# Splitting the weights once per layer, short GpSimd pieces, and a softplus correction without GpSimd

## The reference

```python
kv = np.einsum('bhsd,bhse->bhde', k, v)          # batch 4, heads 8, 576 tokens, 64
out = np.einsum('bhsd,bhde->bhse', q, kv)
rms = np.sqrt(np.mean(out * out, axis=-1, keepdims=True) + 1e-06)
x = (out / rms * g_norm)                         # then as 2304 tokens x 512

h = x @ w_in                                     # 512 x 2048
g = h * (1.0 / (1.0 + np.exp(-1.702 * h)))       # layer 1
x = g @ w_out                                    # 2048 x 512

h = x @ w_in2
g = np.maximum(h, 0.0) + np.log1p(np.exp(-np.abs(h)))   # layer 2: softplus
y = g @ w_out2
```

## Time and profile before

| | us |
|---|---|
| median of 3 runs | 1026.78 (1023.02 to 1027.03) |
| the profiled execution | 1023.06 |
| its span, first to last instruction | 1021.3 |
| mean granted clock of PE | 0.931 of 2.4 GHz |
| PE busy | 868.1 (85%) |
| DVE busy | 698.9 (68%) |
| POOL busy | 540.9 (53%) |
| ACT busy | 433.8 (42%) |
| DMA | 53.28 MB, mean 52 GB/s |

### The profile page before, as it was taken

How to read it: one execution, slowest core, us unless ns; L and a number is a source line. 1 busy time by engine, 2 the same in 40 slices (tenths; PEclk the granted TensorE clock), 3 DMA queues, 4 the chain that set the end, 5 groups by cost and what they waited for, 6 DMA issues and landing times.

```text
span 1021.3 us, 12292 instructions
## 1 busy us (share of the span) xinstructions
PE 868.1 (85%) x4584; PEld 774.1 (76%) x4584; DVE 698.9 (68%) x1029; ACT 433.8 (42%) x751; POOL 540.9 (53%) x416
## 2 busy tenths in 40 slices
...
DMA packets 22219, 53.28 MB, mean 52 GB/s; under 512 B 2064, under 2 KB 7824, under 8 KB 22160
## 3 DMA queue, kind: packets, MB, share of 16 engines
...
q10 hardware_dynamic: 576, 0.33, 0.1%
...
## 4 chain that ended last, share of the span: by engine, by line
DVE 36%; PE 35%; ACT 10%; POOL 8%; issue 7%; DMA 3%; DVEq 0%; POOLq 0%; ACTq 0%
PE ps L514 19%; DVE gs_f L879 9%; PE ps L553 8%; POOL fix L378 8%; DVE gs_f L848 5%; PE ps L556 4%; ACT gs L675 4%; DVE gs L883 4%; DVE xs L812 3%; DVE xs_f L801 3%; DVE gs_f L856 3%; PE ps L559 3%; DVE fix L867 3%; DVE gs_f L875 2%; DMA kv_in_sb<-k_v 2%
## 5 line engine op out<-in xcount | busy, mean ns | idle before, releaser
L514 PE MATMUL ps<-xs,w_in 128*128 128x384 f32 x2016 | 443.1, 363 | 126.1 <-DVE gs_f L848 111.8
L514 PEld LDWEIGHTS ps<-xs,w_in 128*128 128x128 f32 x2016 | 380.8, 205 | 161.3 <-issue 101.5
L357 POOL TENSOR_TENSOR w_in<-w_in_f,w_in 128x1024 fp32r<-128x1024 f32 x96 | 217.2, 2268 | 75.4 <-ACT w_in L680 75.2
L559 PE MATMUL ps<-w_out,gs 128*128 128x512 f32 x864 | 234.0, 409 | 9.0 <-DVE gs L883 8.7
L378 POOL TENSOR_TENSOR fix<-ex,fix 128x384 f32<-128x384 f32 x96 | 111.5, 1161 | 216.8 <-DVE fix L867 216.8
L553 PE MATMUL ps<-gs,w_out 128*128 128x512 f32 x576 | 209.1, 396 | 0.0
L559 PEld LDWEIGHTS ps<-w_out,gs 128*128 128x128 f32 x864 | 168.4, 199 | 43.8 <-issue 16.0
L848 DVE TENSOR_TENSOR gs_f<-ps,gs_f 128x384 f32<-128x384 f32 x240 | 130.8, 550 | 90.6 <-PE ps L514 89.1
L556 PE MATMUL ps<-gs,w_out 128*128 128x256 f32 x576 | 162.8, 283 | 0.0
L879 DVE TENSOR_TENSOR gs_f<-gs_f,fix 128x384 f32<-128x384 f32 x96 | 96.5, 1005 | 61.8 <-POOL fix L378 61.1
L883 DVE TENSOR_TENSOR gs<-gs_f,gs 128x384 fp32r<-128x384 f32 x96 | 91.2, 950 | 52.4 <-ACT gs L675 50.1
...
## 6 DMA issues: line engine op xcount, KB each, us to landing
w_in_f<-w_in SPq DMA_DIRECT2D x48, 512.0 KB, 3.3
kv_in_sb<-k_v SPq DMA_DIRECT2D x16, 512.0 KB, 8.7
w_out_f<-w_out SPq DMA_DIRECT2D x16, 512.0 KB, 4.1
...
tail_sb<-k_v SPq DMA_DIRECT2D x3, 256.0 KB, 11.8
...
```

The source lines that it names most:

```text
L357: nc.gpsimd.tensor_tensor(w[:, LO, slots], w_in32[:, n % W_BUFS, LO, slots], w[:, HI, slots].bitcast(F32), ALU.subtract).then_inc(w_split, 1)
L514: mm = nc.tensor.matmul(ps[:, bank, 0:HALF], w[:, wp, W_OF[k], cols], xs[:, k, xp, t], start=(new and t == 0 and (wp, xp) == (HI, HI)), st ...
L559: mm = nc.tensor.matmul(ps[:, ACC_BANK + j, 0:DM], g[:, j * P:(j + 1) * P], w, start=new, stop=done)
```

## The change

Three things are changed. The split weights of w_in are made once for each of the 16 blocks and written to a scratch in DRAM (`w_kept`, 1.835 MB a block); steps 8 to 47 load their finished operands from there into two of the three buffers, and the third is used to split the eight blocks of the second layer during steps 7, 9, ..., 21. POOL makes all LO parts in pieces of 256 columns. And the correction of the softplus is (1+e)-1-e, made by an added ACT instruction (1+e, of which the logarithm is taken too) and one DVE instruction. Beside these, POOL makes all seven x blocks of the first chunk, and the raw weights of the first three steps are loaded earlier in the attention stage.

```diff
+        w_kept = nc.dram_tensor("w_kept", (2 * STEPS, P, 2 * 7 * KW), F32, kind="Internal").ap()
...
+        def split_buffer(d):
+            return d % W_BUFS if d < STEPS else W_BUFS - 1
+        def raw_loads(d):
+            return d // W_BUFS + 1 if d < STEPS else (STEPS - 1) // W_BUFS + d - STEPS + 1
+        def w_buffer(n):
+            return n % W_BUFS if n < STEPS else n % 2
+        def operand_loads(n):
+            return 3 + (n - STEPS) // 2 + 1
+        def split_at(m):
+            if W_POOL <= m + 2 < STEPS:
+                return m + 2
+            if m >= STEPS - 1 and (m - STEPS + 1) % 2 == 0 and m - STEPS + 1 < 2 * STEPS:
+                return STEPS + (m - STEPS + 1) // 2
+            return None
...
+        X_EARLY = (B11, B21, T2, T3, T4, T1, B22)
...
-            def load_w_in(n):
-                if n >= W_BUFS:
-                    sp.wait_ge(prod_done, PRODUCTS * (n - W_BUFS + 1))
-                src = (w_in1 if n < PHASE1 else w_in2)[n % STEPS]
-                sp.dma_start(w_in32[:, n % W_BUFS, LO, 0:4].rearrange("p a n -> p (a n)"), src
-                             ).then_inc(w_in_landed[n % W_BUFS], 16)
+            def load_raw(d):
+                b = split_buffer(d)
+                if d >= W_BUFS:
+                    last = d - W_BUFS if d < STEPS else STEPS - W_BUFS if d == STEPS else None
+                    if last is not None:
+                        sp.wait_ge(prod_done, PRODUCTS * (last + 1))
+                    sp.wait_ge(w_stored, 16 * ((last if last is not None else d - 1) + 1))
+                sp.dma_start(w_in32[:, b, LO, 0:4].rearrange("p a n -> p (a n)"),
+                             (w_in1 if d < STEPS else w_in2)[d % STEPS]).then_inc(w_in_landed[b], 16)
+            def keep(d):
+                sp.wait_ge(w_split, 7 * (d + 1))
+                sp.dma_start(w_kept[d], w_in[:, split_buffer(d)].bitcast(F32).rearrange("p a s n -> p (a s n)")
+                             ).then_inc(w_stored, 16)
+            def load_operands(n):
+                d = n % STEPS + (0 if n < PHASE1 else STEPS)
+                sp.wait_ge(prod_done, PRODUCTS * (n - 1))
+                sp.wait_ge(w_stored, 16 * (STEPS if n < PHASE1 else d + 1))
+                sp.dma_start(w_in[:, w_buffer(n)].bitcast(F32).rearrange("p a s n -> p (a s n)"), w_kept[d]
+                             ).then_inc(w_in_landed[w_buffer(n)], 16)
...
-            W_AT = {6: 0, 10: 1, 14: 2}
+            W_AT = {3: 0, 8: 1, 13: 2}
...
+            keep(0)
             for m in range(ALL):
-                if m + W_BUFS < ALL:
-                    load_w_in(m + W_BUFS)
+                if m + W_BUFS < STEPS:
+                    load_raw(m + W_BUFS)
+                if m + 1 < STEPS:
+                    keep(m + 1)
+                if STEPS <= m + 2 < ALL:
+                    load_operands(m + 2)
+                if split_at(m) and split_at(m) >= STEPS:
+                    keep(split_at(m))
+                if split_at(m + 1) and split_at(m + 1) >= STEPS:
+                    load_raw(split_at(m + 1))
...
-            def w_low(n, slots):
-                w = w_in[:, n % W_BUFS]
-                nc.gpsimd.tensor_tensor(w[:, LO, slots], w_in32[:, n % W_BUFS, LO, slots], w[:, HI, slots].bitcast(F32),
-                                        ALU.subtract).then_inc(w_split, 1)
-            def w_all(n):
-                w_sums(n)
-                w = w_in[:, n % W_BUFS]
-                nc.gpsimd.tensor_copy(w[:, HI], w_in32[:, n % W_BUFS, LO]).then_inc(w_hi_early, 1)
-                pool.wait_ge(w_hi_early, n + 1)
-                w_low(n, slice(0, 4))
-                w_low(n, slice(4, 7))
+                pool.wait_ge(w_summed, 4 * d + 4)
+            def w_low(d):
+                w, w32 = w_in[:, split_buffer(d)], w_in32[:, split_buffer(d)]
+                for slot in W_OF:
+                    nc.gpsimd.tensor_tensor(w[:, LO, slot], w32[:, LO, slot], w[:, HI, slot].bitcast(F32),
+                                            ALU.subtract).then_inc(w_split, 1)
+            def w_all(d):
+                w_sums(d)
+                b = split_buffer(d)
+                nc.gpsimd.tensor_copy(w_in[:, b, HI], w_in32[:, b, LO]).then_inc(w_hi_early, 1)
+                pool.wait_ge(w_hi_early, d + 1)
+                w_low(d)
...
+                for f in (2 * pair, 2 * pair + 1):
+                    for cols in (slice(0, DM // 2), slice(DM // 2, DM)):
+                        nc.gpsimd.tensor_tensor(w_out[:, f, LO, cols], w_out32[:, f, LO, cols],
+                                                w_out[:, f, HI, cols].bitcast(F32), ALU.subtract
+                                                ).then_inc(w_out_split, 1)
...
-            def softplus_fix(m, tile):
-                i = TILES * (m - PHASE1) + tile
-                pool.wait_ge(back_made, i + 1)
-                nc.gpsimd.tensor_tensor(fix[:, i % 2], ex[:, i % 2], fix[:, i % 2], ALU.subtract
-                                        ).then_inc(fix_made, 1)
...
+            for slot in X_EARLY[2:]:
+                if slot == T2:
+                    pool.wait_ge(x_raw_made, x_raws(0, T4))
+                x_early(slot)
             w_all(1)
             w_all(2)
             w_out_low(0)
-            for m in range(1, ALL + 1):
-                if m > PHASE1:
-                    softplus_fix(m - 1, C12)
-                if m == ALL:
-                    break
-                n = m + 2
-                if W_POOL <= n < ALL:
-                    w_sums(n)
-                if m >= PHASE1:
-                    softplus_fix(m, C11)
-                if W_POOL <= n < ALL:
-                    pool.wait_ge(w_hi_made, n - W_POOL + 1)
-                    w_low(n, slice(0, 4))
+            for m in range(1, ALL):
+                d = split_at(m)
+                if d:
+                    w_sums(d)
+                    pool.wait_ge(w_hi_made, d - W_POOL + 1)
+                    w_low(d)
                 if w_out_of(m):
                     w_out_low(m)
-                if m >= PHASE1:
-                    softplus_fix(m, C21)
-                if W_POOL <= n < ALL:
-                    w_low(n, slice(4, 7))
-                if m >= PHASE1:
-                    softplus_fix(m, C22)
...
-                    pe.wait_ge(w_split, 2 * m + 2)
+                    if m < STEPS:
+                        pe.wait_ge(w_split, 7 * (m + 1))
+                    else:
+                        pe.wait_ge(w_in_landed[w_buffer(m)], 16 * operand_loads(m))
...
+                        act.wait_ge(soft_made, i1 - 1)
                     nc.scalar.activation(ex[:, i % 2], h, ACT.Abs).then_inc(abs_made, 1)
                     act.wait_ge(abs_made, i1 + 1)
                     nc.scalar.activation(ex[:, i % 2], ex[:, i % 2], ACT.Exp, scale=-1.0).then_inc(exp_made, 1)
                     act.wait_ge(exp_made, i1 + 1)
-                    nc.scalar.activation(lg[:, i % 2], ex[:, i % 2], ACT.Ln, bias=1.0).then_inc(log_made, 1)
+                    nc.scalar.activation(fix[:, i % 2], ex[:, i % 2], ACT.Identity, bias=1.0).then_inc(one_more, 1)
+                    act.wait_ge(one_more, i1 + 1)
+                    nc.scalar.activation(lg[:, i % 2], fix[:, i % 2], ACT.Ln).then_inc(log_made, 1)
...
-                if W_POOL <= m + 2 < ALL:
-                    round_w_in(m + 2)
+                if split_at(m):
+                    round_w_in(split_at(m))
...
-                if 0 <= u - 2 * PAIRS - 4 < 4:
-                    low_x(0, X_FIRST_ORDER[u - 2 * PAIRS - 4])
-            low_x(0, B22)
...
-            def back(m, tile):
-                i = TILES * (m - PHASE1) + tile
-                dve.wait_ge(exp_made, i + 1)
-                nc.vector.tensor_scalar(fix[:, i % 2], ex[:, i % 2], 1.0, -1.0, ALU.add, ALU.add
-                                        ).then_inc(back_made, 1)
             def softplus(m, tile):
                 i = TILES * m + tile
                 i1 = i - TILES * PHASE1
                 low = hid(m, tile)
+                dve.wait_ge(one_more, i1 + 1)
+                nc.vector.scalar_tensor_tensor(out=ex[:, i % 2], in0=fix[:, i % 2], scalar=-1.0, in1=ex[:, i % 2],
+                                               op0=ALU.add, op1=ALU.subtract).then_inc(fix_made, 1)
                 dve.wait_ge(log_made, i + 1)
                 nc.vector.scalar_tensor_tensor(out=low, in0=hidden_of(m, tile), scalar=0.0, in1=lg[:, i % 2],
                                                op0=ALU.max, op1=ALU.add).then_inc(hid_read, 1)
                 dve.wait_ge(hid_read, i + 1)
                 dve.wait_ge(fix_made, i1 + 1)
-                nc.vector.tensor_tensor(low, low, fix[:, i % 2], ALU.add).then_inc(soft_made, 1)
+                nc.vector.tensor_tensor(low, low, ex[:, i % 2], ALU.subtract).then_inc(soft_made, 1)
```

More of the change, by code:

```diff
@@ L137, in build @@
         x_made = sem("x_made")
+        w_stored = sem("w_stored")
         w_summed = sem("w_summed")
@@ L157, in build @@
```

(64 more changed lines are left out.)

24 lines of the change are left out of this document (6 added, 18 removed).

## The result

The changed kernel takes 972.25 us (median of 4: 971.99 to 979.29) against 1024.9 before (also of 4, one more than in the table above); the ratio is 0.950, 95% interval 0.946 to 0.955. Predicted were 957, in a range of 930 to 985. The profiled execution is the 979.29 of the four, its span 977.5; the three others lie 7 us lower, so the trace has a few us that the median does not have.

What follows compares the result with a forecast made beforehand. PE was taken to wait for DVE, whose operations with two SBUF inputs wait for GpSimd's instruction in flight. Terms summing to -67.4 took the profiled 1023.06 us to 955.7, raised to 957; range 930 to 985.

Steps and rivals of the forecast that it cites:

- 17 ordinary second-layer steps: Second-layer steps 25 to 30, 33 to 38, 41 to 45: GpSimd's blocks go, 20.36 falls to 17.6 each, -47 us.
- steps 46, 47, end: Last two steps and last down projection: only the chain's 0.65 per step and a little gained, -2 us.
- start to the end of step 0: DVE loses five low x operations to GpSimd, attention units shorten, w_out splits collide more: -4 us.
- steps 1 to 5: First layer: the long block goes, four w_out pieces at 0.42 us take its place, 0 net.
- steps 18, 20, 22: First-layer steps without a split: 17.05 falls to the 15.6 floor as w_out's pieces come early, 1.45 us each.
- 9, 11, 13, 17, 19, 21, clock in it: First-layer split steps: late raw weights make pieces collide with DVE's gates, +10.4 us, plus +4 for the slow clock.
- steps 7, 8, 15, 16: First-layer steps 7, 8, 15 and 16: a small gain, -1 us together.
- rival 2: Second layer: slow clock stays, P1 and P6 remain at 3.87 us; kernel 976 us, chance 0.15.
- 3.2 + 7.8 + 0.6 + 5.95: Ordinary second-layer step: to C22's low part, PE's queue to P4's end, C21's add and signal, C21's Abs to next P1.
- rivals 3: Operand loads in 40 steps arrive late, 30 us each; kernel slower at 1480 us, chance 0.03.
- 4: Rival: GpSimd is not what stretches DVE's operations; about 0.8 us gained a step, kernel 1005 us, chance 0.03.
- Rival 1: First-layer split steps: GpSimd's pieces do not collide with DVE, six steps stay at 15.6; kernel 938 us, chance 0.17.

Runs made afterwards that it cites:

- idle subtractions: Changed kernel with two unused GpSimd subtractions (1024 and 768 columns) in the spare buffer in each step from 26 on: 1039.6 us, ratio 1.016.
- raw weights first: Changed kernel with the next split's raw weights issued on SP's queue before the operands, not behind them: 958.2 us, ratio 0.937.
- idle fills: Changed kernel with two GpSimd fills of 3584 columns, which only write the spare buffer, in each step from 26 on: 972.65 us, ratio 0.951.
- the queue's order: Changed kernel with SP's queue ordered raw weights, w_out, operands, store, GpSimd's order unchanged: 944.8 us, ratio 0.923.

## Why the prediction was right, and where it was not

The forecast of 957 was 15 us too low. The measured 972 lies inside the range of 930 to 985, which was made wide for two rivals that did not come. Span against span (1021.3 and 977.5) the terms came out so (the -5.8 for steps 6, 18, 20 and 22 is in two lines):

| term | predicted | measured |
|---|---|---|
| 17 ordinary second-layer steps | -47 | -48.5 |
| steps 31+32, 39+40 | -17 | -14.2 |
| steps 23+24 | -5 | -6.5 |
| steps 46, 47, end | -2 | +1.3 |
| start to the end of step 0 | -4 | -4.6 |
| steps 1 to 5 | 0 | +5.3 |
| step 6 | -1.5 | -1.5 |
| steps 18, 20, 22 | -4.4 | +1.2 |
| 9, 11, 13, 17, 19, 21, clock in it | +14.4 | +14.4 |
| steps 10, 12, 14 | 0 | +2.0 |
| steps 7, 8, 15, 16 | -1 | +7.3 |
| sum | -67.4 | -43.8 |

*What bounds, and the second layer: right.* The step of 17.6, made of 3.2 + 7.8 + 0.6 + 5.95, measures 17.54 to 17.57, and the two idle times it holds are 0.48 and 0.87. The idle subtractions show the cause and bring it back. The clock stays at 1.00; rival 2 did not happen, nor did rivals 3 (loads of 7.3 us) and 4. At the changes of chunk steps 31 and 39 are the 24.3 that I had; steps 32 and 40 are 24.48 and 23.78 for 22.7.

*But the reason within it was half right.* I counted the correction's removal to the step (the chain with ACT's fourth operation). Measured, the old one does a little better, 17.38. In its trace the wait for GpSimd lies mostly beside ACT's work on C22, so that ACT is idle for only 0.64 before it rounds C21, while the new one puts 0.56 more on ACT for each of the two tiles. The bound I gave from the step at 972.38, 17.76, was the sign.

*First-layer split steps: right in its parts, lucky in its sum.* The raw weights landed 8.3 us after issue, I had 8.0. DVE's gates of C21 and C22 in step 11:

```profile
279.87 0.84 DVE L888 TENSOR_TENSOR gs_f<-gs_f,lg 128x384 f32<-128x384 f32 x1 [0.36 <-ACT lg L697]
280.75 0.78 DVE L891 CAST gs<-gs_f 128x384 fp32r<-128x384 f32 x1
...
282.46 1.09 DVE L888 TENSOR_TENSOR gs_f<-gs_f,lg 128x384 f32<-128x384 f32 x1
```

All six together pay 2.46 us, 2.5 predicted. In the six steps PE is idle 13.7 us in all (14.9 by my 4 x 2.2 and 2 x 3.05) and busy 5.1 more than at 15.60 a step (4 for the clock). But the single steps run from 17.89 to 19.83 where I had 17.8 and 18.65: that the sum meets 14.4 to the tenth is luck. Rival 1 did not happen, but raw weights first make it come true in steps 11, 13 and 17 (15.94, 15.64, 15.61).

*The step that failed* is "7, 8, 15, 16: -1". I had worked out that raw weights land 6.2 after P1 and that ACT rounds them at 9.2, and used it only for the ordinary split steps. In steps 7 and 15 ACT rounds three blocks of x behind this, before the sigmoid of C21, and DVE and PE wait for all of it: +7.3 for -1, and raw weights first took back 4.6 and 4.2 in steps 7 and 15. It did so by starting x's roundings 9.8 us after the start of step 7 and not 14.3. Against the kernel before, though, these roundings are no later (14.6 and 12.6 before in steps 7 and 15, 14.3 and 12.3 after), because there DVE's x operations had been stretched by long GpSimd instructions. The late raw weights ate the gain that was due there. The rest is the second thing that I left out here: the low pieces, pushed back by the same wait, stand beside DVE's row behind the roundings, 8.2 and 7.1 us for 4.9 in both steps before.

*Steps 18, 20, 22*: "w_out's pieces come early" was wrong by the same omission. I named w_out behind the operands for 19 and 21 only; it holds for all (8.8 us to landing for 4.1), and the queue's order brings 18, 20 and 22 to the 15.6 predicted.

*Steps 1 to 5 and the start*: the start's -4 came, and step 1 gave it back, 22.66 for 18.18. PE waited at P1 of step 1 for the second split and then for w_out's low part, the first 12 matmuls at the slow clock (3.86):

```profile
77.45 3.86 PE L549 MATMUL ps<-xs,w_in 128*128 128x384 f32 x12 [5.21 <-POOL w_in L403]
84.39 0.79 PE L588 MATMUL ps<-gs,w_out 128*128 128x512 f32 x1 [3.08 <-POOL w_out L418]
```

I said that GpSimd's splits would be "up to 8 us later" and priced what DVE pays, not that PE waits for them. With DVE's low parts back the kernel with the new queue is 4 faster.

*Step 47*: -2 came out as +1.3, and it is the clock. The last 36 matmuls take 11.24 us here, at a granted clock of 0.74; in the run with the idle fills, behind the same 2.81 us of idle, they take 8.41 at 1.00.

```profile
962.29 11.24 PE L594 MATMUL ps<-w_out,gs 128*128 128x512 f32 x36 [2.81 <-DVE gs L913]
```

```profile
959.17 8.41 PE L605 MATMUL ps<-w_out,gs 128*128 128x512 f32 x36 [2.81 <-DVE gs L924]
```

*Which part of the change earned it*: not as the terms suggested. Kept weights alone give 34, short pieces alone 32, both together 51 to 52, the correction nothing. So the two overlap: each takes long blocks out of the second layer. I had thought that short pieces are no gain. In the kernel before they cost 0.2 us in a first-layer step with w_out's low part (17.26 for 17.06) and win in the second layer; in the changed kernel, where long pieces meet three operations in a row, they win 21.

The 2 us of steps 10, 12 and 14 are a debt of the split steps in front of them: with the raw weights first all three take 15.6. Step 12 begins at the slow clock (3.73 for 12 matmuls behind 2.54 of idle).

Most of the 7 us between the profiled execution and the others can be placed by the run with the idle fills, the same program up to step 26, with a span of 971.5. Of the 6.0 us between the two, 2.8 lie in the last 36 matmuls shown above and 4.6 in steps 20 to 24; the rest nearly cancels.

What stays open is what decides about the clock: the same P1 of step 12 takes 2.32 us behind 2.71 of idle in that run, and 3.73 behind 2.54 here. My estimate of the clock's part went by the length of the idle just before; this pair shows that it does not settle it.
